# Another order for the first pair of heads, and the last output group in two parts, in a fused attention, expert and gated kernel

## The reference

```python
def reference(...):                       # B=2, 8 heads, S=768, head size 64
    # 1 windowed attention: keep the first 4 keys and the 128 newest
    a = softmax(where(is_sink | in_window, q @ k.T / 8, -1e9)); x = a @ v
    # 2 experts: causal attention per expert, weighted by the two best gates
    out = sum(w[e] * softmax(causal(q_e @ k_e.T / 8)) @ v_e @ wo[e])
    # 3 gated layer
    u, vv = split(gelu(x @ w_in)); v_n = layernorm(vv) * g_ln
    v_s = einsum("ts,bsd->btd", w_sg, v_n) + b_sg
    return x + (u * v_s) @ w_out
```

## Time and profile before

| what | value |
|---|---|
| median of the runs | 373.2 us (372.88 to 373.82) |
| the profiled execution | 374.25 us, of which the span is 372.5 us |
| TensorE matmul busy | 363.9 us (98% of the span) |
| VectorE, ScalarE, GpSimd busy | 212.8, 193.0, 142.8 us |
| bytes moved | 24.20 MB, mean 65 GB/s |

### The profile page before, as it was taken

One profiled execution on the slowest core, in us unless ns is written; L12 is line 12 of the kernel. 1 busy time (PEld: TensorE's weight loads), 2 busy tenths in 40 slices (PEclk: granted clock), 3 DMA queues, 4 the chain that ended last, 5 costly groups with the idle time before them and its releaser, 6 DMA issues.

```text
span 372.5 us, 7796 instructions
## 1 busy us (share of the span) xinstructions
PE 363.9 (98%) x2838; PEld 334.7 (90%) x2838; DVE 212.8 (57%) x612; ACT 193.0 (52%) x518; POOL 142.8 (38%) x188
## 2 busy tenths in 40 slices
PE   8799999999999999999999999999999999999996
PEld 6578888889998889999988998899999988999996
DVE  3977776621688883078898608534744265325342
ACT  3999999933789673377888353432311033411110
POOL 4799888897826027000545617410000032100000
PEclk9999999999999999999999999999999999999999
DMA  7746656333320000000231202000011200000112
GB/s 237 223 140 201 190 192 188 106 112 114 114 57 1 4 1 2 2 0 2 56 87 36 91 33 56 2 0 3 0 42 45 84 2 0 0 2 0 45 41 85
DMA packets 12885, 24.20 MB, mean 65 GB/s; under 512 B 1328, under 2 KB 6704, under 8 KB 12848
## 3 DMA queue, kind: packets, MB, share of 16 engines
q1 hardware_dynamic: 12848, 23.70, 20.4%
HBM read 20.55 MB, written 3.15 MB: 64 GB/s over the span
## 4 chain that ended last, share of the span: by engine, by line
PE 92%; DVE 3%; issue 2%; ACT 2%; DMA 1%; SPq 0%; DVEq 0%; ACTq 0%
PE banks L1025 15%; PE banks L1027 15%; PE banks L1026 15%; PE banks L1296 14%; PE banks L1067 6%; PE banks L1110 6%; PE banks L1079 6%; PE banks L1195 5%; PE banks L1231 5%; PE banks L1207 4%; PE banks L1121 2%; DMA qd<-in_qT 1%; DVE Pa L740 1%; ACT Pb L620 1%; PE banks L1211 0%
## 5 line engine op out<-in xcount | busy, mean ns | idle before, releaser
L564 ACT ACTIVATE Pa<-Pa,NMa 128x260 f32<-128x260 f32 (+1 forms) x96 | 46.2, 482 | 10.5 <-DVE NMa L740 10.5
L469 POOL TENSOR_TENSOR Pa<-Pa,RIa 128x520 f32<-128x520 f32 (+1 forms) x48 | 42.7, 909 | 10.9 <-DVE RIa L765 10.9
L740 DVE CUSTOM_DVE_ANT_0 Pa<-banks,win 128x260 f32<-128x260 f32 (+1 forms) x96 | 33.5, 402 | 18.9 <-PE banks L1067 18.6
L545 POOL TENSOR_TENSOR rstd<-vare,minus_half 128x1 f32<-128x1 f32 x12 | 11.9, 990 | 77.6 <-DVE vare L960 77.6
L620 ACT ACTIVATE Pb<-Pb,NM 128x384 f32<-128x384 f32 (+5 forms) x48 | 31.8, 664 | 6.2 <-DVE NM L821 6.0
L720 ACT ACTIVATE gH<-uT 128x384 fp32r<-128x384 f32 x16 | 8.4, 525 | 50.0 <-DVE uT L979 50.0
L821 DVE CUSTOM_DVE_ANT_0 Pb<-banks,causal 128x384 f32<-128x384 f32 (+5 forms) x48 | 28.3, 620 | 7.8 <-PE banks L1195 4.1
L1296 PE MATMUL banks<-w_sgL,vnH 128*128 128x384 f32 x96 | 32.5, 338 | 0.0
L977 DVE TENSOR_TENSOR vb<-banks,b_all 128x384 f32<-128x384 f32 x16 | 8.9, 557 | 37.0 <-PE banks L1296 37.0
L1067 PE MATMUL banks<-kd,qd 64*128 64x260 f32 (+1 forms) x192 | 27.6, 411 | 2.5 <-DVE NMa L740 2.1
L1067 PEld LDWEIGHTS banks<-kd,qd 64*128 64x128 f32 x192 | 17.1, 200 | 10.0 <-issue 7.2
(11 more groups left out here) (153 smaller groups left out, 1078.4 us busy)
## 6 DMA issues: line engine op xcount, KB each, us to landing
va<-in_v SPq DMA_DIRECT2D x8, 384.0 KB, 3.6
out<-raw SPq DMA_DIRECT2D x16, 192.0 KB, 1.9
kd<-in_kT SPq DMA_DIRECT2D x7, 396.0 KB, 5.0
qd<-in_qT SPq DMA_DIRECT2D x7, 384.0 KB, 6.1
vs<-in_vsink SPq DMA_DIRECT2D x8, 336.0 KB, 4.3
raw<-in_w_sgT SPq DMA_DIRECT2D x9, 256.0 KB, 2.8
raw<-in_w_in SPq DMA_DIRECT2D x8, 256.0 KB, 2.7
raw<-in_w_b SPq DMA_DIRECT2D x8, 193.0 KB, 4.6
```

Source lines behind the costliest of these rows:

```text
L469: nc.gpsimd.tensor_tensor(Pa[s][:, h, ts, :], Pa[s][:, h, ts, :], RIa[:, s, h, ts].unsqueeze(2).broadcast_to((P, ts.stop - ts.start, WIN)) ...
L564: nc.scalar.activation(Pa[s][:, h, t, a:WIN], Pa[s][:, h, t, a:WIN], ACT.Exp, bias=NMa[:, s, h, t:t + 1], scale=-1.0, accum_out=RSa[:, s, ...
L740: nc.vector.tensor_tensor_reduce(out=Pa[s][:, h, t, a:WIN], in0=banks[:, score_banks(p, t)[h], 0:WIN - a], in1=m[:, :], scale=-SCALE, scal ...
```

## The change

It does two things. First, the lists of the first pair are written anew on all four engines. Tiles 0 and 1 are scored first, then 3, 4, 2 and 5, and only then the six tiles of the next pair, in the order 0, 2, 1, 4, 5, 3; the groups are scaled and turned beginning with group 0. The lists hold the same steps as before, with other banks, and `A_ACT` copies the same two groups.

Second, the last of the sixteen output groups is made in two parts, of 256 and of 128 columns (`LAST_PARTS`). Each part has its own twelve matmuls, its own addition and its own store. The second part uses bank 0 of `U_BANKS`. The final wait counts one more store.

```diff
-A_PE = [order("s0.1.5 s3.3.2 s1.4.0 s2.1.5 s4.3.2 n1.4.0 n2.1.5 s5.0.4 n3.3.2 n5.0.4 n0.1.5 n4.3.2 t1.1.1 t1.0.0 t0.1.3 t2.0.2 k5 t0.0.0 t2.1.4"),
+A_PE = [order("s0.0.5 s1.2.3 s3.4.0 s4.1.5 s2.0.4 s5.2.3 n0.0.5 n2.0.4 n1.2.3 n4.1.5 n5.2.3 n3.4.0 t0.0.2 t1.1.3 t1.0.4 t0.1.2 k0 t2.0.1 t2.1.3"),
...
-A_ACT = [order("s0 s3 s2 s1 s4 n1 s5 n3 n0 n5 n4 n2 c2.1 c0.0"),
+A_ACT = [order("s0 s1 s3 s2 s5 s4 n0 n2 n1 c0.0 n5 n3 n4 c2.1"),
...
-A_DVE = [order("s0 s3 s1 s2 s4 i1 n1 n2 i0 s5 n3 i2 n0 n5 n4 c1.0 c1.1 k c2.0 c0.1 j"),
+A_DVE = [order("s0 s1 s3 s4 i0 s2 s5 n0 i1 n2 n1 i2 n5 n3 n4 c1.1 c1.0 c0.1 c2.0 k j"),
...
-A_POOL = [order("c1.0 c1.1 c0.0 c0.1 c2.0 c2.1 k l"),
+A_POOL = [order("c0.0 c0.1 c1.0 c1.1 c2.0 c2.1 k l"),
...
+LAST_PARTS = [(0, 2 * P), (2 * P, HALF)]
...
-                sp.wait_ge(s_["o_ready"], n + 1)
-                sp.dma_start(out[row:row + P, g * HALF:(g + 1) * HALF], O[n % 2][:, 0:HALF]).then_inc(stored[n % 2], 16)
+                for i, (a, z) in enumerate(LAST_PARTS if n + 1 == B * MIX_N else [(0, HALF)]):
+                    sp.wait_ge(s_["o_ready"], n + 1 + i)
+                    sp.dma_start(out[row:row + P, g * HALF + a:g * HALF + z], O[n % 2][:, a:z]).then_inc(stored[n % 2], 16)
...
-                wait("down", n + 1)
...
+                for i, (a, z) in enumerate(LAST_PARTS if n + 1 == B * MIX_N else [(0, HALF)]):
+                    wait("down", n + 1 + i)
+                    nc.vector.tensor_tensor(O[n % 2][:, a:z], banks[:, U_BANKS[0] if i else D_BANKS[n % 2], 0:z - a],
+                                            X2[:, n // MIX_N, m, g * HALF + a:g * HALF + z], ALU.add).then_inc(s_["o_ready"], 1)
...
+                for i, (a, z) in enumerate(LAST_PARTS if n + 1 == B * MIX_N else [(0, HALF)]):
+                    if i:
+                        wait("gelu_u", B * MIX_N)
+                    at = slice(g * HALF + a, g * HALF + z)
+                    three(banks[:, U_BANKS[0] if i else D_BANKS[n % 2], 0:z - a], parts(w_outH, w_outL, slice(m * P, (m + 1) * P)),
+                          [(gH[g][:, d, a:z], gL[:, d, at]) for d in range(KT)]).then_inc(s_["down"], 1)
```

More of the change, by code:

```diff
@@ L409, in _ @@
                 row = n // MIX_N * DM + m * P
-                sp.wait_ge(s_["o_ready"], n + 1)
-                sp.dma_start(out[row:row + P, g * HALF:(g + 1) * HALF], O[n % 2][:, 0:HALF]).then_inc(stored[n % 2], 16)
-            for s in range(2):
-                sp.wait_ge(stored[s], 16 * B * MIX_N // 2)
+                for i, (a, z) in enumerate(LAST_PARTS if n + 1 == B * MIX_N else [(0, HALF)]):
+                    sp.wait_ge(s_["o_ready"], n + 1 + i)
+                    sp.dma_start(out[row:row + P, g * HALF + a:g * HALF + z], O[n % 2][:, a:z]).then_inc(stored[n % 2], 16)
+            sp.wait_ge(stored[0], 16 * B * MIX_N // 2)
+            sp.wait_ge(stored[1], 16 * (B * MIX_N // 2 + len(LAST_PARTS) - 1))
         @block.gpsimd
@@ L990, in finish @@
                 g, m = MIXES[n % MIX_N]
-                wait("down", n + 1)
                 if n >= 2:
                     dve.wait_ge(stored[n % 2], 16 * (n // 2))
-                nc.vector.tensor_tensor(O[n % 2][:, 0:HALF], banks[:, D_BANKS[n % 2], 0:HALF], X2[:, n // MIX_N, m, g * HALF:(g + 1) * HALF], ALU.add)\
-                    .then_inc(s_["o_ready"], 1)
+                for i, (a, z) in enumerate(LAST_PARTS if n + 1 == B * MIX_N else [(0, HALF)]):
+                    wait("down", n + 1 + i)
+                    nc.vector.tensor_tensor(O[n % 2][:, a:z], banks[:, U_BANKS[0] if i else D_BANKS[n % 2], 0:z - a],
+                                            X2[:, n // MIX_N, m, g * HALF + a:g * HALF + z], ALU.add).then_inc(s_["o_ready"], 1)
             dve.wait_ge(small_in, 16)
@@ L1308, in down @@
                 wait("o_ready", n - 1)
-                at = slice(g * HALF, (g + 1) * HALF)
-                three(banks[:, D_BANKS[n % 2], 0:HALF], parts(w_outH, w_outL, slice(m * P, (m + 1) * P)),
-                      [(gH[g][:, d, :], gL[:, d, at]) for d in range(KT)]).then_inc(s_["down"], 1)
+                for i, (a, z) in enumerate(LAST_PARTS if n + 1 == B * MIX_N else [(0, HALF)]):
[4 more added lines that the diff above has]
+                          [(gH[g][:, d, a:z], gL[:, d, at]) for d in range(KT)]).then_inc(s_["down"], 1)
             pe.wait_ge(s_["zeros"], 1)
```

## The result

The kernel after takes 371.93 us (median of nine, 371.49 to 372.31); the kernel before took 373.83 us beside it (372.88 to 374.83). The ratio is 0.9949, 95% interval 0.9937 to 0.9962. The forecast was 373.0 with a range down to 372.0. The sign was right, the size was not: −1.9 us instead of −0.15. In absolute time the miss looks smaller than it is, by the luck of the starting point: the forecast went out from 373.2, the median of three runs that are the first three of the nine, and the nine have 373.83.

A forecast was written before the change was run, and what follows sets the result against it. TensorE was taken as the bound, holding 92% of the chain. Start −0.25 us plus end +0.1 us gave −0.15 us, from the median 373.2 to 373.0 us; range 372.0 to 374.4, forecast's chance 0.47.

The forecast's parts named there:

- The start's −0.25 us: First pair's new lists: the net gain taken for the start, bounds −0.7 and +0.3 us.
- the pace until 9 us: TensorE's start: a 260-column pass for both heads costs 0.43 us, a tile 0.87, until the faster pace near 9 us.
- The difference on the median: Whole kernel: profiled execution 374.25 us, 1.05 over the median 373.2; the forecast difference was applied to the median, giving 373.0.
- Bank waits of 0.55 and 0.65: VectorE, first pair: two new idle waits replace two locked inversions and the late start, so VectorE gains only 0.2 us.
- The hold on the token j: Pair 1's inversion: GpSimd holds it from 19.2 to 20.13 us, leaving only 0.15 of the 0.6 us gain.
- the rival that the start keeps its gain: Start: j is not held and values' 0.7 us earlier start passes on, giving 372.6 us; chance 0.10.
- From the last mask to the values: First pair: the last mask ends at 16.66 us and values begin at 18.03 instead of 18.72.
- the gathering is no longer late: GpSimd, first pair: its last two scalings start at 14.07 us and the gathering ends at 16.5 instead of 17.65.
- TensorE's waits near 11.2 and 13.7: TensorE, start: waits for masks of about 1 us each, named as a sign of the predicted course.
- 0.115 us forecast for a 128-column matmul: Last output group, second part: price of each float32r matmul, taken from the one-pass transposes' 0.112 us.
- +0.1 us forecast for the split: Last output group in two parts: the end comes at 372.61 us against 372.5.
- both bounds, 0.062 and 0.226: Short matmul prices: columns only (372.4 us, chance 0.14) or plain float32 (374.3 us, chance 0.23).

The follow-up runs named there:

- no warming up: Kernel after and kernel before, each without any matmul ahead of the first scores (`WARM_UP = 0`): 372.88 us for the new lists, 374.05 for the old.
- without the addition: Small add of 1e-9 to the attention sums left out, reciprocal kept: kernel before 373.67 us (ratio 1.0005), kernel after 372.95 us (ratio 0.9985).
- third profile: Kernel before, unchanged, run again for its profile alone: 373.03 us, quick start, first values at 17.93 us.
- Tile 1's place alone: Kernel before with only tile 1 of the first pair moved right behind tile 0: 373.29 us, ratio 0.9997.
- tile 1 held back: Kernel after, but tile 1 of the first pair waits for the second transfer again: 372.88 us, ratio 0.9978.
- the filled kernel: Kernel before with six matmuls that nobody reads set into the first pair's TensorE list, behind two tiles of the next pair: 373.36 us, ratio 0.9996.

## Why the prediction was wrong, by its steps

**The start's −0.25 us: the term that failed, and first in it the pace until 9 us.** The lists alone measured −1.7 us in the median (371.95 for 373.64). The walk took the slow pace of the earlier trace rows for a property of the program. It was one of two that the kernel before has. In the six profiles in which tile 1 follows tile 0 directly behind six or seven matmuls of warming up, the pace was quick by 6.6 us at the latest. Of the seven in which TensorE stands for the second transfer instead, it stayed slow until about 9 us in three. That the order does this is a correlation over thirteen profiles; what decides it in a single execution the runs do not show. The cost can be read along VectorE's masks: the first wide mask was forecast for 6.16 and came at 5.24, tile 0 of the next pair for 10.77 and came at 9.35. So 1.42 us of the 1.69 us by which the masks ended sooner than forecast (14.97 for 16.66) were there by 9.35 us. At the forecast's own pace the walk ends about right: with no warming up the first tile of the second transfer is begun at 5.38 and the values came at 17.27; the forecast begins it at 5.92 (5.05 and 0.87), which would put the values near 17.8, for the forecast 18.03. That shift is argued, not measured. But the gain was larger at this pace too: 1.32 us between the two kernels without warming up, part of it the wait of 1.16 us, where the walk had 0.7.

**The difference on the median.** The prediction set the profiled 374.25 against 373.2 and "put the difference on the median". The table shows that the profiled execution was of the slow kind. The price of a slow start behind seven matmuls of warming up differs between the lists (0.8 to 1.1 us for the old, 0.4 in the one such profile of the new), so it could not be carried over unchanged.

**Bank waits of 0.55 and 0.65: too large.** They are 0.18 and 0.18 as the profile counts them. From the mask of the next pair's tile 0 to the last mask's end the forecast had 5.89 us, and it took 14.97 − 9.35 = 5.62. That is 0.27 us. The prediction rightly saw that in the new lists bank waits take the place of the locks, and set the two nearly equal, for a gain of VectorE of 0.2 us. Measured without the addition, the locked additions cost the old lists 0.9 us and the new ones nothing, since there the bank wait shrinks by what the lock takes.

**The hold on the token j: wrong.** It was to be held from 19.2 to 20.13 by a GpSimd instruction and to eat 0.45 of 0.6 us. The exponentials were over at 17.6, and the addition took 0.21 us at 17.68. GpSimd in the kernel after:

```profile
17.04 0.82 POOL L458 TENSOR_TENSOR wbH<-raw,ones 128x386 fp32r<-128x386 f32 x1
17.94 0.87 POOL L461 TENSOR_TENSOR wbL<-raw,wbH 128x386 fp32r<-128x386 f32 x1
```

It met the last 0.2 us of one strip instruction and was through before the next. So the 0.45 us that the term −0.25 had set aside for it was not lost. A meeting of two streams that are both 1 us away from their forecast place cannot be called; the rival that the start keeps its gain (0.10) was the nearest to what happened, and still 0.7 us short.

**What was right.** From the last mask to the values 1.37 us were forecast and 1.43 measured; from there to the next pair's scores 1.12 and 1.06. That two bank waits take the place of locked additions, and that the gathering is no longer late, showed as told. TensorE's waits near 11.2 and 13.7, of about 1 us each, came at 9.75 and 12.13 with 0.77 and 0.79. And the end: 0.115 us forecast for a 128-column matmul and 0.112 measured, +0.1 us forecast for the split and +0.05 measured. The transposes were the right neighbour; both bounds, 0.062 and 0.226, were wide of it. The Trainium skill's 107 ns for a load of 128 weights, an estimate from its formula (TensorE: Matmul & The Clock Gate, "LDWEIGHTS (loading the stationary operand)"), agrees with it as a floor. The same page of the Trainium skill under "Back-to-back issue gap" gives about 81 ns for a stream of loads and matmuls of 128 columns; no row here is that short, the measured price is 0.112. One sum of the rivals is slightly off: by the prediction's own terms the split outweighs the −0.25 us from 0.13 us a matmul on, not from 0.14.

**Where the gain comes from, then.** Quick execution against quick execution, the old lists (third profile) against the new ones (lists alone), the first masks of both starting at 5.25. Against tile 0, the first wide mask comes 0.67 us sooner (5.68 for 6.35). The additions last 1.07 instead of 1.60 us in sum. Two waits of 0.2 us for exponentials are gone. Against that, bank waits put 0.27 and 0.26 us behind the reciprocals, and one later mask waits 0.05. That makes −1.0 us, and the masks end 0.95 earlier (15.12 for 16.07). The turning starts 1.08 earlier (13.61 for 14.69) and takes 2.94 instead of 3.24 us: values 1.38 us earlier. Tile 1's place alone brings nothing (ratio 0.9997), and in the new lists its early start is worth 0.3 to 0.5 us. The additions with their locks are a large part: leaving them out brings the values of the old lists 0.9 us earlier and those of the new ones not at all, and the medians of the two are then 0.7 us apart instead of 1.7. The parts overlap, so they do not add up to the whole. In medians the quick executions of before stand 1.06 us above the new lists; the whole of them 1.69 (373.64 for 371.95). The other 0.6 us is that 57 of 96 old executions belong to the slower group or fell to half clock, and the new lists lose little that way. How many of them began slowly is inferred from their times, and why an execution begins slowly stays open.

## What to carry to other kernels

Before an early stretch is walked with the prices of one profile, see whether these prices belong to the program: a tile that costs twice as much before 9 us as after it is a pace, and a second execution may not have it. Where a median stands a full microsecond off the profiled execution, ask which stretch holds that microsecond before forecasting a change in that stretch. The order that keeps TensorE supplied over its first microseconds had its own gain here and, on top, fewer slow executions. And an experiment that removes one wait is read where the wait was before it is read in the total: here 0.9 us won in the first pair was lost again, in a gap right behind it and in a meeting of two engines 100 us later, and the total alone said that the wait had cost nothing.

## What the runs showed of the hardware

The granted clock is shown as 1.00 throughout the first 10 us of an execution whose passes are 0.43 us apart there, and of one whose passes are 0.22 apart; at the start the distance of two matmuls tells the pace and the clock column does not. Later falls do show in it (0.50 from 14 to 16 us above). They came in 22 of 96 executions of the old lists, in 5 of 12 and 6 of 12 of two variants with holes of over 1.1 us near 10 and 13 us, in none of 12 with those holes filled, and in none of the 30 of the new lists, whose holes are of 0.8 us at most. The old lists with the split alone add 3 of 12, the old ones without the addition 0 of 12. Short holes are no warrant, though: the new lists with tile 1 held back have none over 0.8 us either, and 2 of 12 executions fell; nor does a single long one always bring a fall, as the 1.13 us of the filled kernel show. VectorE and GpSimd hold each other up in more than the small additions: a tensor_tensor of 96 columns took 1.10 us instead of 0.25 when GpSimd had begun 0.03 us ahead of it. Float32r matmuls have a floor: 0.175, 0.118 and 0.112 us for 384, 256 and 128 columns, so halving the columns below 256 saves almost nothing. Stores have one too: 192, 128 and 64 KB take 1.9, 1.7 and 1.5 us from issue to landing, which is why splitting the last group could not pay.
